# Token rows fetched per tile instead of scattered into sorted order

## The reference

```python
# 1. linear attention, 8 batches x 8 heads x 576 x 64
kv = einsum('bhsd,bhse->bhde', softmax_over_s(k), v)
x  = einsum('bhsd,bhde->bhse', softmax_over_d(q), kv)      # -> x: 4608 x 512
# 2. soft mixture of experts, 8 experts x 4 slots
logits = x @ phi                                           # 4608 x 32
slot_input = softmax_over_tokens(logits).T @ x
slot_out[e] = relu(slot_input[e] @ w1[e]) @ w2[e]          # F = 1024
x = softmax_over_slots(logits) @ slot_out                  # c (4608 x 32) times 32 x 512
# 3. top-1 mixture of experts
e_idx  = argmax(x @ w_gate, axis=1)
gate_w = softmax(x @ w_gate)[e_idx]; eom = sigmoid(x @ w_output_gate)
out[mask] = gate_w * eom[e] * (relu(x[mask] @ v1[e]) @ v2[e])   # for each expert e
```

## Time and profile before

| | |
|---|---|
| median of 3 runs | 612.21 us (611.94 to 612.46) |
| the profiled execution | 612.41 us, span 610.7 us |
| busy: TensorE, its weight loads | 436.4 us (71%), 252.0 us (41%) |
| busy: VectorE, ScalarE, GpSimd | 352.9 us (58%), 193.7 us (32%), 152.6 us (25%) |
| DMA | 107.56 MB, mean 176 GB/s |
| chain that ended last | PE 43%, DVE 22%, issue 13%, DMA 10%, ACT 7%, POOL 2% |

### The profile page before, as it was taken

The page is one execution under the profiler, slowest core; times in us unless marked ns, Lnnn a source line. Parts: engine busy times, 40 slices in busy tenths (PEclk is TensorE's granted clock), DMA queues, the critical chain, the costliest instruction groups (busy, mean ns, idle before and its releaser), DMA issues.

```text
span 610.7 us, 12791 instructions
## 1 busy us (share of the span) xinstructions
PE 436.4 (71%) x4468; PEld 252.0 (41%) x4469; DVE 352.9 (58%) x574; ACT 193.7 (32%) x310; POOL 152.6 (25%) x134
## 2 busy tenths in 40 slices
PE   1588988887475442236544837999999999999931
PEld 0566666664342322215101214545545545545420
DVE  5889999961668556456853553344344344434462
ACT  0366766674243333312412322112112212212220
POOL 2355555550000000000086640111111111111131
PEclk9889999998597766665788876999999999999965
DMA  9959999226970799976891710110110110111100
GB/s 305 389 185 373 384 371 390 80 88 222 374 284 5 270 351 348 391 285 253 332 368 33 284 58 1 52 53 34 52 52 34 52 52 34 52 52 38 48 17 1
DMA packets 44384, 107.56 MB, mean 176 GB/s; under 512 B 4352, under 2 KB 4928, under 8 KB 44352
## 3 DMA queue, kind: packets, MB, share of 16 engines
q1 hardware_dynamic: 38176, 96.92, 43.1%
q0 software_dynamic: 4592, 10.07, 4.5%
q10 hardware_dynamic: 1584, 0.10, 0.2%
HBM read 96.27 MB, written 12.65 MB: 178 GB/s over the span
## 4 chain that ended last, share of the span: by engine, by line
PE 43%; DVE 22%; issue 13%; DMA 10%; ACT 7%; POOL 2%; another core or an unknown queue 1%; SPq 1%; DVEq 0%; POOLq 0%; ACTq 0%
PE banks L1371 31%; DMA kvg<-in_moe_w 5%; DVE big L876 4%; PE banks L1358 3%; DVE big L729 3%; DMA big<-in_k 3%; DVE top L866 3%; ACT big L613 2%; DMA ring<-in_moe_w 2%; DVE big L702 2%; DVE big L715 2%; POOL big L464 1%; PE banks L1133 1%; PE banks L1314 1%; DVE big L721 1%
## 5 line engine op out<-in xcount | busy, mean ns | idle before, releaser
L1371 PE MATMUL banks<-big,work 128*128 x864 | 193.9, 381 | 0.6 <-ACT work L687 0.6
L1371 PEld LDWEIGHTS banks<-big,work 128*128 128x128 f16 x864 | 83.4, 98 | 95.4 <-issue 2.8
L687 ACT ACTIVATE work<-banks 128x512 f16<-128x512 f32 x86 | 46.8, 595 | 188.2 <-PE banks L1358 188.2
L502 POOL DMA_INDIRECT out<-work,out_row x43 | 42.3, 984 | 200.8 <-DVE work L1039 195.0
L1038 DVE COPY out_row<-tok 128x1 int32 (+1 forms) x43 | 6.6, 153 | 124.0 <-PE banks L1371 120.9
L1030 DVE SCALAR_TENSOR_TENSOR work<-banks,work 128x512 f16<-128x512 f32 x86 | 55.2, 683 | 7.6 <-ACT work L687 7.5
L1275 PE MATMUL banks<-ring,side 128*32 128x128 f32 x384 | 19.9, 392 | 41.1 <-DMA ring<-in_moe_w 40.2
L464 POOL TENSOR_TENSOR big<-big 128x1152 f32<-128x1152 f32 x16 | 33.6, 2118 | 57.1 <-DVE big L734 57.1
L486 POOL DMA_INDIRECT sorted_rows<-tok,pos x36 | 37.1, 1031 | 23.9 <-DVE pos L997 14.3
L1099 PE MATMUL banks<-big 64*64 64x128 f32 x1152 | 36.7, 278 | 7.8 <-ACT big L519 5.4
L866 DVE TENSOR_REDUCE top<-kvg 128x1 f32<-128x2048 f32 x12 | 27.3, 2285 | 24.3 <-DMA kvg<-in_moe_w 24.0
(11 more groups left out here) (187 smaller groups left out, 577.0 us busy)
## 6 DMA issues: line engine op xcount, KB each, us to landing
ring<-in_moe_w SPq DMA_DIRECT2D x20, 2048.0 KB
kvg<-in_moe_w SPq DMA_DIRECT2D x12, 1024.0 KB, 7.4
big<-in_k SPq DMA_DIRECT2D x8, 1152.0 KB, 6.6
big<-in_q SPq DMA_DIRECT2D x8, 1152.0 KB, 7.9
big<-in_v SPq DMA_DIRECT2D x8, 1152.0 KB, 9.8
big<-in_moe_w SPq DMA_DIRECT2D x4, 2048.0 KB, 13.8
big<-in_moe_w SPq DMA_DIRECT2D x4, 1024.0 KB, 9.4
sorted_rows<-work SPq DMA_DIRECT2D x1, 731.0 KB, 15.8
```

Source lines behind the costliest of these rows:

```text
L502: pool.indirect_dma_start(out=out, out_offset=bass.IndirectOffsetOnAxis(ap=out_row[:, n:n + 1].bitcast(U32), axis=0), in_=y_out[n], in_off ...
L687: act.activation(h_hi[n][:, b * 512:(b + 1) * 512], psum[2 * n + b], ACT.Relu).then_inc(h_hi_ready, 1)
L1371: return pe.matmul(psum[4 + n], h[n][:, j * P:(j + 1) * P], w_pair[:, ds(ev, 1), w, j, :].rearrange("p o n -> p (o n)"), start=j == 0 and ...
```

## The change

The rows are no longer scattered. `tok`'s rows lose the token's number (ROW = 33) and are written to memory in token order, by one DMA on ScalarE's queue, as soon as the factors are there. What is worked out instead is the inverse of `pos`: for each place in the sorted order the number of its token. Each token number is split into its upper part plus one and its lower six bits (`id_hi`, `id_lo`). In four blocks of nine columns VectorE makes one-hot rows: `row_hot`, 1 where the token's row within its tile is r, and `tile_hot`, `id_hi` and `id_lo` where its tile is n. TensorE multiplies the one with the other and adds up all 36 columns in one PSUM bank (`find_tokens`). Then `hi * 64 + lo` less 64 is the token's number, and a place with nothing in it gets SKIP. The four blocks lie within the rounds 0 to 3 of `g_split_of`, and `token_of` is made behind round 4; the loops of VectorE and TensorE over the rounds are written out.

In the loop over the tiles GpSimd fetches the coefficient rows of tile t + 5 with an indirect DMA behind the store of tile t; `take` waits for its tile's fetch. The store goes by a column of `token_of`, so the copy L1038 is gone. Some small tiles moved into `big`, and the table, its blanking and its load are gone.

```diff
@@ sync
-            sp.wait_ge(table_blank, 2)
-            sp.dma_start(table.rearrange("(p t) w -> p (t w)", p=P), blank).then_inc(table_blanked, 16)
...
-            sp.wait_ge(scattered, 16 * NT)
-            sp.dma_start(tok[:, 0:TILES * ROW], table.rearrange("(p t) w -> p (t w)", p=P)).then_inc(srt_loaded, 16)
-            sp.wait_ge(srt_loaded, 16)
@@ gpsimd
-            scatter(0, AHEAD)
+            pool.wait_ge(table_written, 16)
+            pool.wait_ge(cT_copied, 3)
+            pool.memset(tok[:, 0:TILES * ROW], 0.0).then_inc(rows_cleared, 1)
             for e in range(E):
                 pool.wait_ge(gtop_done, e + 1)
                 pool.partition_all_reduce(top_all[:, :], top[:, :], P, bass.bass_isa.ReduceOp.max).then_inc(
                     gtop_all_done, 1)
-                if e + 1 < E:
-                    scatter(AHEAD + e * (NT - AHEAD) // (E - 1), AHEAD + (e + 1) * (NT - AHEAD) // (E - 1))
+
+            def gather(t):
+                pool.indirect_dma_start(
+                    out=srt[:, t, :], out_offset=None, in_=table,
+                    in_offset=bass.IndirectOffsetOnAxis(ap=token_of[:, t:t + 1].bitcast(U32), axis=0),
+                    bounds_check=N - 1, oob_is_err=False).then_inc(gathered[t % 2], 16)
...
+            pool.wait_ge(token_ready, 1)
+            pool.wait_ge(rows_cleared, 1)
+            gather(0)
+            gather(1)
+            for t in range(2, 5):
+                pool.wait_ge(c_rows_ready, t - 1)
+                gather(t)
             for t in range(TILES):
                 store(t, t % 2)
+                if t + 5 < TILES:
+                    pool.wait_ge(c_rows_ready, t + 4)
+                    gather(t + 5)
@@ scalar
+            act.wait_ge(factor_done, 1)
+            act.wait_ge(c_lo_done, 1)
+            act.dma_start(table.rearrange("(i p c) w -> p i c w", i=NPAIR, c=C),
+                          tok[:, 0:NT * ROW].rearrange("p (i c w) -> p i c w", i=NPAIR, c=C)).then_inc(table_written, 16)
@@ vector
-            dve.memset(blank, 0.0).then_inc(table_blank, 1)
...
+            dve.tensor_scalar(id_part, pos[:, :], 6, None, ALU.logical_shift_right).then_inc(ids_split, 1)
+            dve.tensor_scalar(pos[:, :], pos[:, :], 63, None, ALU.bitwise_and).then_inc(ids_split, 1)
+            dve.wait_ge(ids_split, 2)
+            dve.tensor_scalar(id_hi[:, :], id_part, 1.0, None, ALU.add).then_inc(ids_split, 1)
+            dve.tensor_copy(id_lo[:, :], pos[:, :]).then_inc(ids_split, 1)
...
-            dve.scalar_tensor_tensor(pos[:, :], pos_r[:, :], float(TILES), pos_t[:, :], ALU.mult, ALU.add).then_inc(
-                pos_done, 1)
+            dve.tensor_copy(at_tile, pos_t[:, :]).then_inc(pos_placed, 1)
+            dve.tensor_copy(at_row, pos_r[:, :]).then_inc(pos_placed, 1)
...
+            def one_hots(k):
+                n, part = k % 2, slice(k * TC, (k + 1) * TC)
+                if k >= 2:
+                    dve.wait_ge(token_found, k - 1)
...
+                dve.tensor_tensor(in_tile, over(at_tile, part, TILES), steps_t, ALU.is_equal).then_inc(in_tile_done, 1)
+                dve.tensor_tensor(row_hot[n], over(at_row, part, P), steps_r, ALU.is_equal).then_inc(hot_done, 1)
+                dve.wait_ge(in_tile_done, k + 1)
+                for a, x in ((0, id_hi), (1, id_lo)):
+                    dve.tensor_tensor(tile_hot[n][:, :, a], in_tile, over(x, part, TILES), ALU.mult).then_inc(hot_done, 1)
+                dve.wait_ge(hot_done, 3 * k + 3)
...
-            with dve.Fori(0, E // 2 - 1) as h:
-                g_split_of(2 * h, 0)
-                g_split_of(2 * h + 1, 1)
-            g_split_of(E - 2, 0)
-            g_split_of(E - 1, 1, last=True)
+            for e in range(4):
+                g_split_of(e, e % 2)
+                one_hots(e)
+            g_split_of(4, 0)
+            dve.wait_ge(token_found, 4)
...
+            g_split_of(5, 1)
+            g_split_of(6, 0)
+            g_split_of(7, 1, last=True)
...
+                dve.wait_ge(gathered[n], count)
                 src = srt16[:, ds(t, 1), 0:2 * NS].to_broadcast([P, 2, 2 * NS])
...
-                dve.tensor_copy(out_row[:, n:n + 1], srt[:, ds(t, 1), ROW - 1].bitcast(I32)).then_inc(row_copied, 1)
@@ tensor
+            def find_tokens(k):
+                pe.wait_ge(hot_done, 3 * k + 3)
...
+                for t in range(TC):
+                    last = pe.matmul(psum[6][:, 0:2 * TILES], row_hot[n][:, t, :],
+                                     tile_hot[n][:, t].rearrange("p a n -> p (a n)"),
+                                     start=k == 0 and t == 0, stop=k == 3 and t == TC - 1)
+                last.then_inc(token_found, 1)
...
-            with pe.Fori(1, E // 2 - 1) as h:
+            for h in (1, 2):
+                find_tokens(2 * h - 2)
                 project(2 * h + 1, 1, 16 * h + 16 * (E - 1))
                 fold_up(2 * h, 0)
+                find_tokens(2 * h - 1)
                 project(2 * h + 2, 0, 16 * h + 16 * E)
                 fold_up(2 * h + 1, 1)
```

More of the change, by code:

```diff
@@ L295, in vision_block_kernel @@
         w_split = sem("w_split")
-        scattered = sem("scattered")
-        srt_loaded = sem("srt_loaded")
+        ids_made = sem("ids_made")
+        ids_split = sem("ids_split")
+        pos_placed = sem("pos_placed")
+        in_tile_done = sem("in_tile_done")
+        hot_done = sem("hot_done")
+        token_found = sem("token_found")
+        token_step = sem("token_step")
+        token_ready = sem("token_ready")
+        table_written = sem("table_written")
+        gathered = [sem(f"gathered{n}") for n in (0, 1)]
+        rows_cleared = sem("rows_cleared")
         c_rows_ready = sem("c_rows_ready")
@@ L477, in _ @@
                 reduce_w(e)
-            pool.wait_ge(factor_done, 1)
-            pool.wait_ge(c_lo_done, 1)
-            pool.wait_ge(iota_done, 1)
-            pool.wait_ge(pos_done, 1)
-            def scatter(first, end):
-                for t in range(first, end):
-                    pool.indirect_dma_start(out=table, out_offset=bass.IndirectOffsetOnAxis(
-                        ap=pos[:, t:t + 1].bitcast(U32), axis=0), in_=rows[:, t, :], in_offset=None).then_inc(
-                            scattered, 16)
-            AHEAD = 8
-            scatter(0, AHEAD)
+            pool.wait_ge(table_written, 16)
+            pool.wait_ge(cT_copied, 3)
+            pool.memset(tok[:, 0:TILES * ROW], 0.0).then_inc(rows_cleared, 1)
             for e in range(E):
@@ L1019, in take @@
+            dve.scalar_tensor_tensor(token_of[:, :], found, -64.0, empty, ALU.add, ALU.add).then_inc(token_ready, 1)
+            g_split_of(5, 1)
+            g_split_of(6, 0)
+            g_split_of(7, 1, last=True)
+            def take(t, n, count):
+                dve.wait_ge(gathered[n], count)
                 src = srt16[:, ds(t, 1), 0:2 * NS].to_broadcast([P, 2, 2 * NS])
@@ L1054, in step @@
                 if static is None or static + 3 <= TILES - 1:
-                    take(t + 3, m)
+                    take(t + 3, m, count)
                 if static is None or static + 1 <= TILES - 1:
```

109 lines of the change are left out of this document (59 added, 50 removed).

## The result

| | before | changed kernel |
|---|---|---|
| median (runs of one comparison) | 612.34 us (611.94 to 613.28, 4 runs) | 627.59 us (624.68 to 628.88, 4 runs) |
| ratio | | 1.024 (95%: 1.0202 to 1.0278) |
| profiled execution, its span | 612.41, 610.7 us | 627.18, 625.4 us |
| busy: PE, DVE, ACT, POOL | 436.4, 352.9, 193.7, 152.6 us | 440.3, 360.9, 193.9, 162.5 us |
| granted clock, mean | 0.858 | 0.853 |

What follows compares the result with a forecast made beforehand. TensorE was taken to bound the tile loop, but the stretch from 290 to 366 us, with no engine full, to decide. Stage +13.0, entry +0.1 and tail -0.2 made +12.9 us, so 625 us; 8-in-10 range 616 to 634.

Steps and rivals of the forecast that it cites:

- The sign and the mechanism: Rounds 0 to 3: TensorE and VectorE wait for each other in turn; the kernel gets slower, chance 0.92.
- The four rounds: Rounds 0 to 3 of the folding, with one-hots and token products: 12.15 us each.
- Begin low and end high, and take the middle: TensorE's clock in rounds 0 to 3: between 10.1 us at the upper level and 14.2 at the lower, 12.15 us.
- the upper end of 10.1: Rounds 0 to 3 at the upper clock: 10.1 us each; as a rival, with cheaper one-hots, 617 to 619 us, chance 0.11.
- the second rival: Rounds 0 to 3: TensorE's clock stays low throughout, 14.2 us a round, 633 to 636 us; chance 0.11.
- The entry: Start of the tile loop: take 2 comes 3.2 us after take 0; net of the 0.65 us won, +0.1 us.
- the scatters set the pace of most rounds: Folding rounds of the kernel before: four scatters are 5.1 us of the 6.2 us a round.
- The loop: Loop over the sorted tiles: TensorE stays full at 5.68 us a tile despite a second indirect DMA; counted 0.
- The term for the table's zeroing and write: Start of the kernel: dropping the zeroing and write of the table gives 0 to -1.5 us; taken as 0.
- the write of the rows: Table write on ScalarE's queue, 0.6 MB: covered by slack before the maximum, 0; if that fails, at most +1.5 us.
- the tail: After the loop: fetches have some 3 us spare, counted 0; the removed row-number copy gives -0.2 us.
- it falls into the idle time: Rival, rounds 0 to 3: one-hots fit VectorE's idle time, 6.1 us a round, 601 us; chance 0.06.

Runs made afterwards that it cites:

- filling the wait: Changed kernel with 60 unused matmuls of 128 columns ahead of each of the four groups of token products: 620.32 us, ratio 1.0201 to the kernel before.
- the good order: Changed kernel with token products behind project and fold in TensorE's program: 606.73 us (0.9871), repeated 607.77 us (0.9857); some of its profiles add fetch or cast edits.
- the bad one: The changed kernel's own order, token products ahead of project and fold in TensorE's program: 627.59 us, ratio 1.024 to the kernel before.

## Why the prediction was right, and where it was off

- **The sign and the mechanism** held: TensorE's program order makes the two engines alternate for four rounds. Moving each block's nine small products in TensorE's program, with the same instructions, turns 1.024 into 0.987.
- **The four rounds**: forecast 12.15 us, measured 47.95 us for four, from the end of low half 0 at 316.14 to that of low half 4 at 364.09: 11.99 each. Its terms: one-hots 2.76 (forecast 2.8), token products 0.82 (0.7 to 1.3), project 3.64 and fold 2.79 in one round, 3.34 and 1.98 in another. "Begin low and end high, and take the middle" was right, and filling the wait shows in three rounds that the upper end of 10.1 would have been 9.76. Of the Trainium skill's rule ("TensorE: Matmul & The Clock Gate", section "HAM oscillation — how this bites in real kernels"), a throttle anew in every round, the trace agrees: each of the four projects began at the lower level behind its wait. What did not come is what I had made of it in the second rival, a round at the lower level throughout: the upper one came back within the same burst, and the round cost 12.0, not 14.2 us.
- **Ahead of the rounds** 4.96 us (forecast 5.2), **the last three low halves** 14.73 us (14.2). The stage as a whole: 67.6 us from the first maximum, forecast 68.0.
- **The entry**: take 2 came 3.4 us behind take 0 (forecast 3.2), the sum +0.2 (forecast +0.1).
- **A reading that was wrong**: "the scatters set the pace of most rounds". Five of the eight all-reduces did begin right behind a scatter, but with 28 of the 36 left out five of the seven gaps between maxima stayed as they were. The sum did not rest on it: it went from the measured end of the stage, which has the stray wait in it, and all three profiles of kernels with all the scatters have that wait.
- **The loop** stayed full with two indirect DMAs in each tile. The Trainium skill's 3100 ns beside a VectorE copy ("SBUF — State Buffer", section "A bandwidth-pool intuition that's wrong (but worth ruling out)") did not show: fetches 1027 ns, stores 1015 in the mean, where 984 was the store's before. But the Trainium skill puts that delay down to the copy's own length, and the takes beside these DMAs are copies of 0.2 us, so the rows do not test it for a long copy.
- **Off: the start.** The first maximum came 1.4 us later, where I had counted 0.1. The term for the table's zeroing and write ("0 to -1.5, and I take 0") was right at 0: k(1) was read at 19.30 to 19.70 us in the three profiles of the changed front part with a short cast, and at 19.49 and 19.93 in the two of before's kind. In the profile compared here VectorE came to it only at 21.66, since its cast was held up:

```profile
21.66 4.26 DVE L709 TENSOR_REDUCE big<-big 128x256 f32<-128x2304 f32 x1
```

  That delay alone does not reach the routing, for the cast was long in two of the four profiles with before's front part (first maximum at 307.3 in both) and short in one of the changed kind (310.71). The eight profiles of kernels with the changed front part and no forced order have the first maximum at 310.2 to 312.7 us, the four with the front part of before at 307.3 to 309.8, and the two in which GpSimd waits for the cast at 305.6 and 307.1. So some 3 us upstream seem to belong to the change, of which the pair of profiles compared here shows 1.4. Where they arise is not settled. A candidate that no run takes out is the write of the rows (594 KB, issued at 298.85), beside the loads of v1. From the start of the first `project` to that of the third, which waits for its load, it is 12.4 to 14.5 us in the ten profiles with the write and 11.2 to 11.8 in the four without. The sum had put it at 0 and, if its cover fails, at +1.5.
- **Off: the tail.** "In the tail some 3 spare; I count 0", and -0.2 for the copy: it was +0.7. Three takes waited 2.07, 0.41 and 1.02 us for their fetches, so the 3 us were not there; but these waits were taken up again, since without them the tail was as long (32.6 us); one of 3.78 us in another profile was not (34.5). What is longer is the very end: from the start of the last store to the end of the span it is 8.3 to 8.4 us in all ten profiles with the changed front part, and 7.7 to 7.8 in the three of before with all its stores. What happens there is open. The copy brought nothing.
- Together: +14.7 instead of +12.9 us in the profiled pair, 627.59 instead of 625 in the median. The two small terms I had set to about nothing, start and tail, make up all of the difference (+1.3 and +0.9), and the other terms give back some 0.3.

The account of the stage, in sizes that profiles showed: 41.5 us without one-hots and scatters; 47.1 with eight scatters ahead; 55.05 with all of them and one stray wait (before). With one-hots: 45.5 to 50.5 in the good order, 59.4 in the bad one with the clock held up in three of four rounds, 67.65 in the bad one. Without the scatters the stage was 13.5 us shorter, 5.6 for the eight ahead and 8 for the stray wait and the round behind it; with the profile of 49.0 the one-hots cost 7.5 of it, and the place of nine products 18.6.

## What to carry to other kernels

Work moved onto a second engine is cheap only if its wait stands behind everything that the first engine needs next: write down, for one round, which instruction of each engine waits for which of the other, and look for a cycle that holds all of them. If two engines take turns, first move the waiting instruction back in its program; the lower clock of TensorE is a second, smaller bill on the same idle time. And a rival of the kind "it falls into the idle time" should be tried, even if the written order forbids it: here it was two lines of the program away and worth 3.6%.

## What the runs showed of the hardware that was not expected

**A VectorE cast held for the whole of a GpSimd instruction.** In the changed kernel the cast of 128 step numbers and GpSimd's shift of q begin 0.05 us apart:

```profile
13.28 4.04 POOL L458 TENSOR_TENSOR big<-big 128x2304 f32<-128x2304 f32 x1
```

```profile
13.33 4.07 DVE L790 CAST steps_f<-slot_in 128x128 f32<-128x128 int32 x1 [0.33 <-POOL slot_in L448]
```

In the profile of before the cast came first, by 0.09 us, and took 0.20:

```profile
13.26 0.20 DVE L787 CAST steps_f<-slot_in 128x64 f32<-128x64 int32 x1
```

```profile
13.35 4.05 POOL L457 TENSOR_TENSOR big<-big 128x2304 f32<-128x2304 f32 x1
```

Who is first varies between profiles of the same code: two of three others with before's front part had 4.04 us, and one with the changed code had 0.22. In all nine profiles where GpSimd began first, by 0.05 to 0.06 us, the cast took 4.04 to 4.07, and in the three where the cast began first 0.18 to 0.22. With the wait on GpSimd it was 0.23 in both. The Trainium skill ("SBUF — State Buffer", section "SBUF: two separate sides") says that VectorE, in its two-port modes, and GpSimd lock one pair of ports between them, and that the one that starts first keeps it for its whole instruction. The trace agrees: the cast ends 0.08 us behind GpSimd's instruction, not with its own work. That the cast runs in such a mode the trace does not show. What the 4 us cost at the end is not settled either, as said above.

**Signals of TensorE came late beside dense scatters.** The chain has a wait of 6.05, of 6.17, and of 6.38 and 5.07 us in the three profiles of kernels with all the scatters, the first of each at nearly the same place (328.85, 326.45, 326.37), and none in the eleven of kernels with eight scatters or none. Each time VectorE, which waits for the fold, and ScalarE, which waits for the project, go on within 0.1 us of each other (in the profile of before at 334.92 and 334.98, where the fold's row ends at 329.56). In the loop, where indirect DMAs come in pairs every 5.68 us, it did not come. What it is, the runs don't say; that in these profiles it came only with the scatters they show.

**The kernel before moved with the chip, the changed one, measured twice, did not.** Before: 612.34, 614.14, 606.9 and 614.74 us in four comparisons; the changed kernel 627.59 and 627.34, the second on the chip where before took 606.9. No profile of before was taken on that chip, so whether its stray waits are fewer there stays open.
